# A routed mixture of experts behind an attention recurrence: weight loads told by TensorE's entry into an expert, token places counted in slots, and three groups of fill products around the table

## The reference

```python
attn_out = _attn_ref(q, k, v, a_re, a_im)          # a decaying complex state, 4 x 8 heads, 768 steps
x = attn_out.transpose(0, 2, 1, 3).reshape(3072, 384)
h = x @ w_in                                       # 384 x 2048
x = (max(h, 0) + alpha * min(h, 0)) @ w_out        # 2048 x 384
# routed part, 8 experts of 384 x 1024 x 384
do_compute = x @ w_skip > 0
xc = x[do_compute]
logits = xc @ w_gate
e_idx = argmax(logits); gate_w = softmax(logits)[e_idx]
for e in range(8):
    mask = e_idx == e
    y[mask] = gate_w[mask, None] * (max(xc[mask] @ w1[e], 0) @ w2[e])
out = x.copy(); out[do_compute] = xc + y
```

## Time and profile before

| | |
|---|---|
| median of 3 runs | 837.38 us (836.81 to 839.99) |
| the profiled execution | 844.62 us, span 842.7 us |
| mean granted TensorE clock | 0.955 |
| PE busy / DVE busy / ACT busy | 723.2 / 608.2 / 477.9 us |
| end of the first phase's last product | 664.9 us of the span |
| first product of expert 0 | 691.2 us |
| last product of expert 7 | 837.0 us |

### The profile page before, as it was taken

The page is one execution under the profiler, slowest core; times in us unless marked ns, Lnnn a source line. Parts: engine busy times, 40 slices in busy tenths (PEclk is TensorE's granted clock), DMA queues, the critical chain, the costliest instruction groups (busy, mean ns, idle before and its releaser), DMA issues.

```text
span 842.7 us, 15379 instructions
## 1 busy us (share of the span) xinstructions
PE 723.2 (86%) x5472; PEld 698.4 (83%) x5472; DVE 608.2 (72%) x1251; ACT 477.9 (57%) x937; POOL 53.1 (6%) x56
## 2 busy tenths in 40 slices
PE   1213749999999999999999999999999679799896
PEld 1213749999898999989999899999999579799896
DVE  4987878997997998899799799864333554434343
ACT  8267359579649838946964983843343333323330
POOL 2000000000000000000000000000000113233232
PEclk9999659999999999999999999999999859899999
DMA  5565653346226415615432642361610386814200
GB/s 166 156 194 116 155 155 86 87 104 183 73 66 196 120 48 147 177 43 142 145 86 76 189 117 58 83 180 49 202 66 1 111 319 207 313 35 182 86 27 20
DMA packets 82430, 104.67 MB, mean 124 GB/s; under 512 B 15991, under 2 KB 68385, under 8 KB 82337
## 3 DMA queue, kind: packets, MB, share of 16 engines
q1 hardware_dynamic: 79648, 98.44, 39.3%
q0 software_dynamic: 1792, 3.76, 1.4%
q10 hardware_dynamic: 896, 1.25, 0.7%
HBM read 61.04 MB, written 12.19 MB: 87 GB/s over the span
## 4 chain that ended last, share of the span: by engine, by line
PE 41%; DVE 24%; ACT 14%; issue 8%; SPq 6%; DMA 4%; POOL 0%; ACTq 0%; DVEq 0%; POOLq 0%
PE out_ps L657 9%; PE mlp_ps L2224 9%; PE mlp_ps L645 9%; PE out_ps L2238 6%; SPq L358 2%; ACT sq L925 2%; ACT s_t L957 2%; ACT L886 2%; DVE arena L1339 2%; DVE sq L1349 2%; DMA arena<-in_qk 2%; PE att_ps L576 2%; DVE g L1502 2%; DVE sq L1350 2%; SPq L373 2%
## 5 line engine op out<-in xcount | busy, mean ns | idle before, releaser
L657 PE MATMUL out_ps<-w_out_hi,g_parts 128*128 128x394 f32 x768 | 219.8, 347 | 0.0
L645 PE MATMUL mlp_ps<-xT,w_in_hi 128*128 128x384 f32 x768 | 202.7, 345 | 10.6 <-DVE g L1502 9.6
L645 PEld LDWEIGHTS mlp_ps<-xT,w_in_hi 128*128 128x128 f32 x768 | 137.2, 190 | 17.6 <-DVE g L1502 15.3
L657 PEld LDWEIGHTS out_ps<-w_out_hi,g_parts 128*128 128x128 f32 x768 | 142.1, 188 | 2.6 <-issue 1.8
L657 PE MATMUL out_ps<-w_out_lo,g_parts 128*128 128x394 f32 x384 | 131.1, 341 | 0.0
L645 PE MATMUL mlp_ps<-xT,w_in_lo 128*128 128x384 f32 x384 | 130.0, 339 | 0.0
L963 ACT ACTIVATE bent<-mlp_ps,bend_size 128x384 f32<-128x384 f32 x128 | 73.7, 576 | 88.9 <-PE mlp_ps L645 88.6
L1502 DVE SCALAR_TENSOR_TENSOR g<-mlp_ps,slope_side,bent 128x384 f32<-128x384 f32 x128 | 78.0, 614 | 59.7 <-ACT bent L963 58.9
L971 ACT ACTIVATE g_parts<-g 128x384 fp32r<-128x384 f32 x128 | 66.2, 517 | 52.2 <-PE out_ps L657 49.6
L2293 ACT ACTIVATE hT<-mlp_ps 128x256 fp32r<-128x256 f32 x52 | 19.9, 383 | 100.7 <-PE mlp_ps L2224 100.7
L645 PEld LDWEIGHTS mlp_ps<-xT,w_in_lo 128*128 128x128 f32 x384 | 72.7, 189 | 0.0
(11 more groups left out here) (168 smaller groups left out, 1226.1 us busy)
## 6 DMA issues: line engine op xcount, KB each, us to landing
kq<-qk_dec SPq DMA_DIRECT2D x88, 144.0 KB, 3.0
arena<-in_a SPq DMA_DIRECT2D x24, 384.0 KB, 4.2
arena<-in_qk SPq DMA_DIRECT2D x24, 384.0 KB, 3.3
w_sb<-in_w SPq DMA_DIRECT2D x6, 1536.0 KB, 7.9
w_raw<-in_w SPq DMA_DIRECT2D x6, 1536.0 KB, 11.7
xT<-y_parts SPq DMA_DIRECT2D x48, 144.0 KB, 2.8
arena<-in_w SPq DMA_DIRECT2D x4, 1536.0 KB, 9.4
v_nat<-in_v SPq DMA_DIRECT2D x24, 192.0 KB, 3.5
```

Source lines behind the costliest of these rows:

```text
L645: last = pe.matmul(ps[:, 0:HT], w_in_v[s][:, kk, f * P:(f + 1) * P], xT[n.p][:, kk, m, :], start=(kk == 0 and j == 0), stop=(kk == KT - 1 ...
L657: last = pe.matmul(out_ps[i][:, 0:DL], g_parts[:, f % 4, s, i * P:(i + 1) * P], w_out_v[m][:, f, :], start=(f == 0 and j == 0), stop=(f == ...
```

## The change

Four edits, all in `phase2`:

- **Loads.** SyncE loads only expert 1 ahead of the first gather's landing, and experts 2 and 3 behind it. From expert 4 on, both loads of e first wait until TensorE has counted `expert_begun` up e - 2 times: TensorE's sequencer adds one at the head of each expert's code. So `w2` of expert 4 is issued when TensorE enters expert 1, no longer as soon as its buffer is free.
- **Places counted in slots.** The constants of the two counting products are divided by 128, so that places come out in units of slots. One VectorE instruction over 192 columns goes (`before_pp`'s product now brings the subtraction with it), rounding to a slot number takes one instruction in place of three, adding `dropped` is folded in, and `row_of` is counted in negative 128ths, with `lane_part` (a new ScalarE instruction ahead of `split(0)`) to compare with.
- **Fill products.** Ten stand ahead of the wait for the first group's entries, four ahead of the second group's, none ahead of the third's, and ten behind the table in place of nine.
- Order of some small VectorE copies.

```diff
-            for e in range(1, BODY - 1):
+            load_w1(1)
+            load_w2(1)
+            sp.wait_ge(x_gathered, 16)
+            for e in range(2, BODY):
                 load_w1(e)
                 load_w2(e)
-            sp.wait_ge(x_gathered, 16)
-            load_w1(BODY - 1)
-            load_w2(BODY - 1)
             for e in range(BODY, EXPERTS):
+                sp.wait_ge(expert_begun, e - BODY + 2)
                 load_w2(e)
                 load_w1(e)
...
+            def idle_products(n):
+                for _ in range(n):
+                    pe.matmul(att_ps[2][:, 0:NT * EXPERTS], before_pp[:, :], members, start=True, stop=True)
+
+            before_group = [10, 4, 0]
             for t in range(NT):
                 if t % GROUP == 0:
+                    idle_products(before_group[t // GROUP])
                     pe.wait_ge(entries_made, t // GROUP + 1)
...
             last.then_inc(table_full, 1)
-            for _ in range(9):
-                pe.matmul(out_ps[1][:, 0:NT * EXPERTS], before_pp[:, :], members, start=True, stop=True)
+            idle_products(10)
...
+                pe.sem_inc(expert_begun, 1)
                 with pe.If(n > 0):
                     slot(is_first=True)
...
+            act.wait_ge(index_cast, 4)
+            act.activation(lane_part[:, :], lane[:, :], ACT.Copy, scale=-1.0 / P).then_inc(lanes_scaled, 1)
             split(0)
...
+            dve.tensor_scalar(dropped_far[:, :], dropped[:, :], WHOLE, None, ALU.add).then_inc(far_made, 1)
             dve.wait_ge(exp_made, 1)
...
-            dve.tensor_tensor(flat(place), sums[:, :], mlp_ps[1][:, 0:NT * EXPERTS], ALU.subtract).then_inc(step, 1)
+            dve.tensor_tensor(flat(place), sums[:, :], mlp_ps[0][:, 0:NT * EXPERTS], ALU.add).then_inc(step, 1)
...
-            dve.tensor_tensor(flat(place), flat(place), mlp_ps[0][:, 0:NT * EXPERTS], ALU.add).then_inc(step, 1)
...
-            dve.tensor_tensor(dest[:, :], dest[:, :], dropped[:, :], ALU.add).then_inc(step, 1)
-            dve.wait_ge(step, 20)
-            dve.tensor_scalar(slot_of[:, :], dest[:, :], 1.0 / P, -(P - 1.0) / (2 * P), ALU.mult, ALU.add).then_inc(step, 1)
-            dve.wait_ge(step, 21)
-            dve.tensor_scalar(slot_of[:, :], slot_of[:, :], WHOLE, None, ALU.add).then_inc(step, 1)
-            dve.wait_ge(step, 22)
-            dve.tensor_scalar(slot_of[:, :], slot_of[:, :], -WHOLE, None, ALU.add).then_inc(step, 1)
-            dve.wait_ge(step, 23)
-            dve.scalar_tensor_tensor(out=row_of[:, :], in0=slot_of[:, :], scalar=-float(P), in1=dest[:, :],
-                                     op0=ALU.mult, op1=ALU.add).then_inc(rows_known, 1)
+            dve.wait_ge(far_made, 1)
+            dve.scalar_tensor_tensor(out=slot_of[:, :], in0=dest[:, :], scalar=-(P - 1.0) / (2 * P), in1=dropped_far[:, :],
+                                     op0=ALU.add, op1=ALU.add).then_inc(step, 1)
+            dve.wait_ge(step, 19)
+            dve.scalar_tensor_tensor(out=row_of[:, :], in0=slot_of[:, :], scalar=-WHOLE, in1=dest[:, :],
+                                     op0=ALU.add, op1=ALU.subtract).then_inc(rows_known, 1)
...
-            pool.memset(ones_pp[:, :], 1.0).then_inc(triangles, 1)
-            pool.memset(before_pp[:, :], 1.0).then_inc(index_made, 1)
+            pool.memset(ones_pp[:, :], 1.0 / P).then_inc(triangles, 1)
+            pool.memset(before_pp[:, :], 0.0).then_inc(index_made, 1)
```

More of the change, by code:

```diff
@@ L2061, in phase2 @@
         lane = sb("lane", [P, P])
+        lane_part = sb("lane_part", [P, P])
+        dropped_far = sb("dropped_far", [P, NT])
         slot_of = sb("slot_of", [P, NT])
@@ L2097, in phase2 @@
         distance = sem("distance")
+        lanes_scaled = sem("lanes_scaled")
+        far_made = sem("far_made")
         table_full = sem("table_full")
@@ L2107, in phase2 @@
         expert_left = sem("expert_left")
+        expert_begun = sem("expert_begun")
         x_gathered = sem("x_gathered")
@@ L2265, in _ @@
             for t in range(NT - GROUP, NT):
-                act.activation(far_off[:, t + GROUP - NT, :], lane[:, :], ACT.Abs, bias=row_of[:, t:t + 1], scale=-1.0).then_inc(distance, 1)
+                act.activation(far_off[:, t + GROUP - NT, :], lane[:, :], ACT.Abs, bias=row_of[:, t:t + 1], scale=1.0 / P).then_inc(distance, 1)
             act.wait_ge(distance, GROUP)
-            act.activation(in_row[:, NT - GROUP:NT, :], far_off[:, :, :], ACT.Relu, bias=1.0, scale=-1.0).then_inc(late_rows_made, 1)
+            act.activation(in_row[:, NT - GROUP:NT, :], far_off[:, :, :], ACT.Relu, bias=1.0, scale=-float(P)).then_inc(late_rows_made, 1)
             def place_x(s):
@@ L2363, in _ @@
-            dve.tensor_tensor(flat(place), flat(place), mlp_ps[0][:, 0:NT * EXPERTS], ALU.add).then_inc(step, 1)
+            dve.tensor_copy(gate_hi[:, :], gate[:, :]).then_inc(step, 1)
             dve.wait_ge(step, 11)
-            dve.tensor_tensor_scan(slot_sums[:, :], ones_pp[:, 0:EXPERTS], slots[:, :], 0.0, ALU.mult, ALU.add).then_inc(step, 1)
-            dve.tensor_copy(gate_hi[:, :], gate[:, :]).then_inc(step, 1)
+            dve.tensor_tensor_scan(slot_sums[:, :], goes_on[:, 0, 1:EXPERTS + 1], slots[:, :], 0.0, ALU.mult, ALU.add).then_inc(step, 1)
@@ L2367, in _ @@
+            dve.tensor_copy(slots_i[:, 0:EXPERTS], slots[:, :]).then_inc(step, 1)
             dve.wait_ge(step, 13)
             dve.tensor_tensor(base[:, :], slot_sums[:, :], slots[:, :], ALU.subtract).then_inc(step, 1)
-            dve.tensor_copy(slots_i[:, 0:EXPERTS], slots[:, :]).then_inc(step, 1)
+            dve.tensor_copy(slots_i[:, EXPERTS:], slot_sums[:, EXPERTS - 1:EXPERTS]).then_inc(slots_known, 1)
             dve.wait_ge(step, 15)
-            dve.scalar_tensor_tensor(out=place[:, :, :], in0=base[:, :].unsqueeze(2).broadcast_to([P, EXPERTS, NT]),
-                                     scalar=float(P), in1=place[:, :, :], op0=ALU.mult, op1=ALU.add).then_inc(step, 1)
@@ L2373, in _ @@
-            dve.tensor_copy(slots_i[:, EXPERTS:], slot_sums[:, EXPERTS - 1:EXPERTS]).then_inc(slots_known, 1)
+            dve.tensor_tensor(place[:, :, :], place[:, :, :], base[:, :].unsqueeze(2).broadcast_to([P, EXPERTS, NT]), ALU.add).then_inc(step, 1)
+            dve.tensor_copy(factor[:, :, 1], gate_hi[:, :].bitcast(F32)).then_inc(factor_made, 1)
+            dve.wait_ge(step, 16)
+            dve.tensor_tensor(place[:, :, :], place[:, :, :], member[:, :, :], ALU.mult).then_inc(step, 1)
+            dve.tensor_tensor(factor[:, :, 2], gate[:, :], gate_hi[:, :].bitcast(F32), ALU.subtract).then_inc(factor_made, 1)
@@ L2374, in _ @@
             dve.wait_ge(step, 17)
-            dve.tensor_tensor(place[:, :, :], place[:, :, :], member[:, :, :], ALU.mult).then_inc(step, 1)
-            dve.tensor_copy(factor[:, :, 1], gate_hi[:, :].bitcast(F32)).then_inc(factor_made, 1)
+            dve.tensor_reduce(out=dest[:, :], in_=place[:, :, :].rearrange("p e t -> p t e"), op=ALU.add, axis=AX.X).then_inc(step, 1)
             dve.wait_ge(step, 18)
-            dve.tensor_reduce(out=dest[:, :], in_=place[:, :, :].rearrange("p e t -> p t e"), op=ALU.add, axis=AX.X).then_inc(step, 1)
@@ L2404, in _ @@
                                   factor[:, at, :].unsqueeze(3).broadcast_to(parts), ALU.mult).then_inc(entries_made, 1)
-            last_step = 23
+            last_step = 19
             def keep_x(s):
@@ L2494, in _ @@
             pool.tensor_copy(e_index[:, :], e_index_i[:, :]).then_inc(index_cast, 1)
-            pool.memset(ones_pp[:, :], 1.0).then_inc(triangles, 1)
-            pool.memset(before_pp[:, :], 1.0).then_inc(index_made, 1)
+            pool.memset(ones_pp[:, :], 1.0 / P).then_inc(triangles, 1)
+            pool.memset(before_pp[:, :], 0.0).then_inc(index_made, 1)
             pool.memset(goes_on[:, :, :], 1.0).then_inc(scan_set, 1)
             pool.wait_ge(index_made, 2)
-            pool.affine_select(out=before_pp[:, :], in_=before_pp[:, :], compare_op=ALU.is_gt, fill=0.0, base=0,
+            pool.affine_select(out=before_pp[:, :], in_=before_pp[:, :], compare_op=ALU.is_gt, fill=-1.0 / P, base=0,
                                pattern=[[1, P]], channel_multiplier=-1).then_inc(triangles, 1)
```

10 lines of the change are left out of this document (5 added, 5 removed).

## The result

| | before | after |
|---|---|---|
| median | 841.03 us (18 runs, 836.81 to 845.16) | 833.92 us (18 runs, 830.54 to 836.76) |
| ratio | | 0.9908, 95% interval 0.9892 to 0.9925 |
| profiled execution | 844.6 us, span 842.7 us | 833.9 us, span 832.1 us |
| mean granted clock | 0.955 | 0.965 |

The kernel is 7.1 us faster, 0.9%. The forecast was 13.2 us, 1.6%: the direction was right and the size about twice too large. The three runs shown ahead of the forecast had a median of 837.4 us, 18 runs 841.0. So the 833.9 us stand at the very end of the range of 816 to 834. Ratios leave out slow runs, which here are two: one of 1077.9 us of the kernel with places in slots, one of 850.2 us of the kernel before.

What follows compares the result with a forecast made beforehand. Bound by dependent steps up to expert 0's first product, then TensorE with stops for instruction packets among the experts. Terms summed to -14.7 us on the profiled 844.6; nine tenths, -13.2 on 837.4, gave 824.2 us, range 816 to 834.

Steps and rivals of the forecast that it cites:

- Term A: Up to expert 0: shorter VectorE steps, full clock at the table and a faster gather start the transposes 4.0 us earlier.
- Rival 2: At the table: clock still low, fill products delay it, A only -1.0, about 827 us in all; chance 0.10.
- Term B: Into expert 2: with loads held back, the branch out of expert 1 finds DMA engines all but idle; -5.5 us.
- Rival 1: Branch out of expert 1: loads are not what delays the instruction fetch; about 829 us in all; chance 0.12.
- Term C: Into expert 5: moved code removes the second stop for an instruction packet and the half clock; -3.5 us.
- Rival 3: Experts' code: packet edges don't move as counted, so the gains at experts 4 to 7 stay away; 829 us; chance 0.12.
- Terms D and E: Moved code shortens stops: ahead of experts 4 and 6 by 1.2 us together, ahead of expert 7 by 0.8 us.
- Expert 1's +0.3: Expert 1's head now has only 20 instructions to a packet's edge: 0.3 us lost, bounds 0 to +4.0.
- nine tenths: Last step: runs are 7.2 us shorter than the profiled execution, so -14.7 us there becomes -13.2 us in the runs.

Runs made afterwards that it cites:

- without the waits: Changed kernel without SyncE's waits for `expert_begun`, so loads from expert 4 on go out once their buffers are free; 0.9954 of the kernel before, 838.0 us.
- with the tiles last: Changed kernel with the new tiles `lane_part` and `dropped_far` allocated behind `hT`; 0.9911 of the kernel before, 834.7 us.
- with late counts: Changed kernel, TensorE reading only expert 0's count ahead of the transposes, each other at its expert's entry; 0.9943 of the kernel before, 837.5 us.
- with 32 bytes more: Changed kernel with 32 more bytes per partition behind the two new tiles, restoring alignment modulo 64; 0.9900 of the kernel before.
- all together: Changed kernel with loads staggered behind gathers, counts read one by one, 15 fill products ahead and 14 behind, new tiles last; 0.9935, 835.5 us.
- kernel with 15 fill products: Changed kernel with 15 fill products instead of 10 ahead of the table's first group; 0.9904 of the kernel before, 833.5 us.
- kernel with moved code: Kernel before with fifteen products (60 instructions) behind a branch not taken, ahead of expert 0; 0.9957 of the kernel before, 838.65 us.
- kernel with one instruction more: Kernel before with a never-taken branch whose body the compiler dropped, leaving one more instruction; 0.9999 of the kernel before, profiled execution 839.2 us.

## Why the prediction was right in direction and wrong in size

**Term A, up to expert 0 (-4.0 forecast; -1.9 measured against before): the step that failed.** VectorE's part was right: row_of is done 0.8 us earlier (0.9 forecast), and the first entries came at 676.89 - 1.07 = 675.8 us against before (675.7 forecast). Wrong was the way from the clock's return to the pause. The text let the clock come back 5.3 us after the counting products begin, "so here by about 673"; it came 3.1 us after them (668.84 to 672.0 of the span), at 670.9 against before. The ten fill products, faster for it, were done at 673.5 against before and not at 674.5, and "the idle 1.2 us before 675.7" became 2.38 us, after which the clock fell. The 1.75 us that this was compared with are no safe length either: in the profile of the fill products alone it fell after 1.66 us. So the table ended 0.7 us earlier instead of 2.4. The gather landed in 3.27 us (3.1 forecast). Then the counts' loads, which start about when the table ends (683.7 us of the span), ended last. Rival 2's mechanism came true in this profile, though A lost less by it than its bound of -1.0 said.

The second half of the failure is that the 4 us were to pass on to the end. The transposes come 25.2 us behind the first phase in the kernel before and 23.3 in the changed one; where the clock stayed up at the same table, without the waits and with the tiles last, 21.0 and 20.9, which is all that A forecast. Yet expert 1's first product comes 47.8 us behind the first phase in the kernel before, 45.9 in the changed one, and 46.2 and 46.0 in those two. In each of them 1.5 to 1.9 us arrive, whatever the table did.

**Expert 0's slots (nothing forecast).** At full clock the first layer took 5.62 us instead of 7.20, a gain of 1.6 that the forecast left out; it expected the clock to fall once more, which it did in those two profiles. The waits for the second and the third gather took 0.9 and 0.6 us of it back. The text checked expert 2's `w2` and the second gather singly; four loads of 1.5 MB behind one event are under way until some 709 us, and the two gathers there took 6.0 and 8.9 us; a later one, under the loads of experts 4 and 5, took 9.0.

**Term B, into expert 2 (-5.5; -5.4): right.** With the second load held back the branch takes 3.47 us and the clock doesn't fall. Rival 1, that loads don't delay the fetch, falls: without the waits alone the branch is back at 6.10 us. The Trainium skill's rule (DMA: Bandwidth & Descriptors, Queues, rings and completion order), round the queues packet by packet, was read in the forecast as a price near nothing, and the runs show up to 4.4 us. They don't show the rule itself to be wrong: the page lets a packet hold up to 64 descriptors, and in the trace expert 5's `w2` moves in 1024 pieces, 64 for each of 16 engines.

**Term C, into expert 5 (-3.5; -2.2): mechanism right, size off.** The second stop is gone, as forecast, and in this profile the low clock too; in those with late counts, with 32 bytes more, with the tiles last and with all together it came back, after stops of 3.64, 3.06, 2.95 and 2.50 us. The text took 1.5 us for the remaining cost and it is 2.56 + 0.26 = 2.8. The loads are not the reason. Expert 7's `w1`, issued at 773.97 us, landed 8.0 us later and so lies over the branch begun at 779.7, but expert 4's lay over the branch out of expert 1 no less, and in both the packet starts 1.04 us after the branch. What differs is a second packet of code moving at the same time: the two take 1.8 and 2.2 us, where one alone takes about 1.0. The kernel with 15 fill products, whose code lies 20 instructions further, separates them. Expert 7's `w1` lies over its fetch as well (landed 2.7 us after the branch began), only one packet moves, and the branch takes 3.50 us, the stop 0.92:

```profile
L2135 PEldq COMPARE_BRANCH  x1: 3504/3504/3504, 780.8 to 780.8; - x1
```

The text looked for packets behind the experts' heads only, so this one was missing from the term. Rival 3, that the edges don't move as counted, falls by the kernel with moved code. With the loads alone it is another matter: there a whole `w1` begins to move 1.7 us ahead of the branch, the packet starts 2.4 us after it, and the two stops make 4.24 us.

**Terms D and E (-1.2 and -0.8; -1.8 and -1.0): right**, D at its good bound: no stop is left ahead of experts 4 and 6. Expert 1's +0.3 didn't show.

**Not in the sum: the second layer.** 4.23 us instead of 4.18, +0.7 us in 13 slots, from where two new tiles lie.

**Adding up.** -1.9 - 5.4 - 2.2 - 1.8 - 1.0 + 0.7 = -11.6, and 1.07 from the first phase: -10.5 us, the difference of the two spans (10.6). The forecast had -14.7 for the same sum; A makes 2.1 of the 3.1 us between them, C 1.3, the second layer 0.7, and D, E and expert 1 give back about 1.1. The remaining step is the last, and it cost more than A: "stops for code may be part of that, so I take nine tenths". The runs gave 7.1 of 10.6, two thirds. The profiled execution of before (844.6 us) lies at the upper end of the 18 runs (841.0 in the middle, 845.2 the longest), and part of its excess probably lies in the stops that the change removes: in the profile of the kernel with one instruction more expert 5 cost 2.4 instead of 4.98 us. A sum read from one execution must pay its discount where that execution is dear.

## What to carry to other kernels

Where much code is jumped over, the place of branch targets in the instruction stream is worth as much as an optimisation (0.4% here for sixty instructions never run), and any edit ahead of them moves it: compare an edit with a version that only shifts the code before believing its own reason. Hold bulk loads back when a fetch or a small gather is about to come, but look at every small transfer behind the event that releases them, since the loads then all lie there. Products that are to keep the clock up must be counted at the clock that they bring back: at 2.4 GHz they end sooner, and a pause follows. They gave nothing here, because the work behind them then waited for transfers.

## What was not expected of the hardware

- Two tiles, 608 bytes a partition together, placed ahead of others, made the second layer's 24 products 4.23 us instead of 4.18 in every slot; allocated last, 4.18 again; with 32 bytes more, 4.23.
- Two packets of instructions moving together take 1.8 and 2.2 us, where one takes about 1.0, and the branch 5.2 us instead of 3.5.
- Ahead of a fetch the rest of one load cost nothing to be seen (the packet started 1.04 us after the branch), a whole load 3.6 to 4.4 us.
- A scatter of 128 rows took 7.4 us to land under 1.5 MB of loads, and through the wait on its address list it held up VectorE for 3.06 us.
- After 2.56 us of standing still ahead of expert 5 the clock stayed at 1.00, and after 2.95 us there it fell; ahead of the table it fell after 2.38 and, with the fill products alone, after 1.66 us, and stayed after 1.5 us in two profiles: the length of a pause alone doesn't tell.
